# Three early routed slots instead of two in a fused mLSTM, dense layer and routed expert kernel

## The reference

```
y = mlstm(q, k, v, i_gate, f_gate, o_gate)        # 4 x 8 heads, 768 steps, head size 40
x = y.transpose(0, 2, 1, 3).reshape(3072, 320)
h = x @ w_in                                       # 320 x 2048
g = where(h >= 1, h, where(h <= -1, 0, (h + 1)**2 / 4))
x2 = g @ w_out                                     # 2048 x 320
logits = x2 @ w_gate                               # 8 experts
e = argmax(logits); gate = softmax(logits)[e]
out[e == i] = gate * (maximum(x2[e == i] @ w1[i], 0) @ w2[i])    # 320 x 1024, 1024 x 320
```

## Time and profile before

| | |
|---|---|
| median of 3 runs | 833.38 us (832.4 to 834.68) |
| the profiled execution | 833.21 us, its span 831.3 us |
| TensorE busy in the span | 767.5 us (92%) |
| VectorE, ScalarE, GpSimd busy | 593.1, 423.6, 317.3 us |
| mean granted TensorE clock | 0.984 of full |

### The profile page before, as it was taken

The page is one execution under the profiler, slowest core; times in us unless marked ns, Lnnn a source line. Parts: engine busy times, 40 slices in busy tenths (PEclk is TensorE's granted clock), DMA queues, the critical chain, the costliest instruction groups (busy, mean ns, idle before and its releaser), DMA issues.

```text
span 831.3 us, 17200 instructions
## 1 busy us (share of the span) xinstructions
PE 767.5 (92%) x5765; PEld 745.5 (90%) x5765; DVE 593.1 (71%) x1006; ACT 423.6 (51%) x649; POOL 317.3 (38%) x297
## 2 busy tenths in 40 slices
PE   2788999999999999999999999888659999999994
PEld 1788999999999999999999999888659999999994
DVE  4554868787887878888878786666376777776850
ACT  3024445454545455454646454554366666676751
POOL 3342543435454454434445444433232323231111
PEclk9999999999999999999999999999889999999998
DMA  7952222222232223222222202356965244627200
GB/s 222 297 153 74 76 90 75 89 79 96 85 99 79 100 92 94 75 89 74 89 74 89 84 6 71 110 163 207 327 212 173 104 133 159 219 77 227 83 20 5
DMA packets 41457, 97.05 MB, mean 117 GB/s; under 512 B 6937, under 2 KB 24481, under 8 KB 39754
## 3 DMA queue, kind: packets, MB, share of 16 engines
q1 hardware_dynamic: 37498, 87.46, 33.1%
q0 software_dynamic: 3920, 9.08, 3.6%
HBM read 105.63 MB, written 9.33 MB: 138 GB/s over the span
## 4 chain that ended last, share of the span: by engine, by line
PE 81%; DVE 7%; issue 4%; DMA 3%; ACT 3%; SPq 1%; POOL 0%; POOLq 0%; DVEq 0%; ACTq 0%
PE bank L1359 22%; PE bank L1371 21%; PE bank L1492 11%; PE bank L1439 7%; PE bank L1314 5%; PE bank L1305 3%; PE bank L1453 3%; PE bank L1322 2%; PE bank L1331 2%; DVE w_l L1045 2%; DVE w_l L1039 1%; DMA wTt<-in_w_outT 1%; DMA raw<-in_w 1%; ACT w_h L723 1%; PE bank L1385 1%
## 5 line engine op out<-in xcount | busy, mean ns | idle before, releaser
L539 POOL TENSOR_TENSOR g_t<-u_t,r_t 128x512 f32<-128x512 f32 x96 | 135.8, 1415 | 252.9 <-ACT u_t L689 252.9
L684 ACT ACTIVATE r_t<-bank,neg 128x512 f32<-128x512 f32 x96 | 66.0, 688 | 184.9 <-PE bank L1359 184.9
L1371 PE MATMUL bank<-wo_h,g_h 128*128 128x328 f32 x384 | 128.6, 335 | 5.9 <-DVE g_l L990 5.9
L1371 PE MATMUL bank<-wo_h,g_l 128*128 128x328 f32 x384 | 121.3, 316 | 0.0
L1371 PE MATMUL bank<-wo_l,g_h 128*128 128x328 f32 x384 | 121.2, 316 | 0.0
L984 DVE TENSOR_SCALAR u_t<-bank 128x512 f32<-128x512 f32 x96 | 66.1, 689 | 76.2 <-ACT r_t L684 46.9
L621 POOL DMA_INDIRECT out_x<-ob,idx_tok x31 | 37.7, 1217 | 171.5 <-ACT ob L759 167.5
L689 ACT ACTIVATE u_t<-u_t,half 128x512 f32<-128x512 f32 x96 | 69.6, 725 | 41.2 <-DVE u_t L984 40.1
L920 DVE TENSOR_TENSOR_SCAN W<-W,cst 128x512 f32<-128x512 f32 x48 | 83.6, 1745 | 3.8 <-DMA W<-decays 3.8
L1371 PEld LDWEIGHTS bank<-wo_h,g_h 128*128 128x128 f32 x384 | 73.4, 191 | 9.1 <-DVE g_l L990 6.6
L1359 PE MATMUL bank<-xT_h,wi_h 128*128 (+1 forms) x384 | 78.8, 287 | 1.6 <-issue 1.6
(11 more groups left out here) (231 smaller groups left out, 1943.1 us busy)
## 6 DMA issues: line engine op xcount, KB each, us to landing
raw<-in_w SPq DMA_DIRECT2D x12, 1280.0 KB
W<-decays SPq DMA_DIRECT2D x24, 512.0 KB, 5.0
raw<-in_w SPq DMA_DIRECT2D x12, 1024.0 KB
raw2n<-in_w SPq DMA_DIRECT2D x7, 1280.0 KB
raw1n<-in_w SPq DMA_DIRECT2D x7, 1024.0 KB
raw<-in_w SPq DMA_DIRECT2D x24, 256.0 KB
qG<-in_q SPq DMA_DIRECT2D x24, 180.0 KB
qT<-in_qt SPq DMA_DIRECT2D x48, 80.0 KB
```

The source lines that it names most:

```text
L539: pool.tensor_tensor(g_t[p % 2][:, :], u_t[p % 2][:, :], r_t[p % 2][:, :], ALU.add).then_inc(sm["g_done"], 1)
L684: act.activation(r_t[p % 2][:, :], bank_h[p % 2][:, :], ACT.Relu, bias=neg1[:, 0:1]).then_inc(sm["r_done"], 1)
L1371: mm = pe.matmul(bank_acc[tt][:, 0:DL], l[p % 4][:, c], r[:, f, :], start=f == 0 and a == 0, stop=f == NT1 - 1 and a == 2)
```

## The change

Slot kinds become PPPH, three times PPH, three times PH (before: five times PPH, twice PH); both have twelve P and seven H slots. `EARLY` is 3. The third early slot's gather and the reading of the early tokens move, and in the last block ScalarE's and VectorE's splits of slot 0's w1 come one piece later. Behind the last block the order on ScalarE, VectorE, TensorE and in SyncE's queue is written anew.

```diff
-KINDS = "PPH" * 5 + "PH" * 2
+KINDS = "PPPH" + "PPH" * 3 + "PH" * 3
-EARLY = 2
+EARLY = 3
@@ sync: last_stores, and behind the blocks
                 store_x2(t)
+                refill(1)
                 refill2(0)
...
-            load_routed(2)
-            load_routed2(2)
-            refill(1)
-            for s in range(2, NS):
+            load_routed(3)
+            refill(2)
+            load_routed2(3)
+            refill2(1)
+            for s in range(3, NS):
                 refill(s)
                 refill2(s - 1)
@@ gpsimd: body
-                    if not att and p == 5:
+                    gated(t, p)
+                    if not att and p == 1:
+                        table_rows(t, 1)
+                    if not att and p == 4:
                         for tt in range(2):
                             pool.wait_ge(x2_st[tt], 16 * t)
                         pool.wait_ge(sm["zrow"], 16)
                         pool.wait_ge(sm["list_done"], 1)
-                        gather(0)
-                    gated(t, p)
-                    if not att and p == 1:
-                        table_rows(t, 1)
-                    if not att and p == 6:
-                        gather(1)
+                    if not att and p in (4, 5, 6):
+                        gather(p - 4)
@@ scalar: body, tail, and behind the blocks (its first part)
-                    if not att and p in (4, 5):
-                        w1_high(0, p - 4)
+                    if not att and p in (5, 6):
+                        w1_high(0, p - 5)
...
                 w2_high(0, 0)
-                w2_high(0, 1)
...
             h_high(0, 0)
+            h_high(0, 1)
             w1_high(1, 0)
-            h_high(0, 1)
+            h_high(0, 2)
             w1_high(1, 1)
-            h_high(0, 2)
             h_high(0, 3)
             y_high(1)
+            w2_high(0, 1)
@@ vector: body and tail
-                        elif p == 5:
+                        elif p == 4:
                             early_tokens()
-                        if p in (5, 6):
-                            w1_low(0, p - 5)
+                        if p in (6, 7):
+                            w1_low(0, p - 6)
...
                 w2_low(0, 0)
-                w2_low(0, 1)
@@ tensor: body and tail
-                    if not att and p == 4:
+                    if not att and p == 3:
                         turn_table(1, bank_dc[:, 128:256], bank_dc[:, 256:384], 2 * EARLY)
...
                 turn_y(1)
                 second2(0, range(0, NT2 // 2))
-                first_wide(1, 0)
+                for p in range(4):
+                    first_wide(1, p)
+                turn_y(2)
                 turn_experts(2, bank_r[:, 256:384], HALVES)
-                for p in range(1, 4):
-                    first_wide(1, p)
-                second2(0, range(NT2 // 2, NT2 - 2))
+                second2(0, range(NT2 // 2, NT2))
+                for p in range(3):
+                    first_wide(2, p)
                 turn_table(2, bank_r[:, 0:128], bank_r[:, 128:256], HALVES)
-                second2(0, range(NT2 - 2, NT2))
+                first_wide(2, 3)
                 second2(1, range(0, NT2 - 2))
-                turn_y(2)
+                turn_y(3)
                 second2(1, range(NT2 - 2, NT2))
-                first2(2)
+                first2(3)
```

More of the change, by code:

```diff
@@ L809, in _ @@
             h_high(0, 0)
+            h_high(0, 1)
             w1_high(1, 0)
-            h_high(0, 1)
+            h_high(0, 2)
             w1_high(1, 1)
-            h_high(0, 2)
             h_high(0, 3)
             y_high(1)
+            w2_high(0, 1)
             h_high(1, 0)
-            w2_high(1, 0)
             h_high(1, 1)
-            w2_high(1, 1)
             h_high(1, 2)
             h_high(1, 3)
+            w1_high(2, 0)
+            y_high(2)
+            w1_high(2, 1)
             act.wait_ge(sm["list_done"], 1)
             out_gate(0)
-            w1_high(2, 0)
-            w1_high(2, 1)
-            y_high(2)
+            h_high(2, 0)
+            w2_high(1, 0)
+            h_high(2, 1)
+            w2_high(1, 1)
+            h_high(2, 2)
+            h_high(2, 3)
             w1_high(3, 0)
             w1_high(3, 1)
+            y_high(3)
+            out_gate(1)
             w2_high(2, 0)
             w2_high(2, 1)
+            w1_high(4, 0)
+            w1_high(4, 1)
+            w2_high(3, 0)
+            w2_high(3, 1)
             act.wait_ge(sm["list_done"], 2)
@@ L1187, in _ @@
             all_blocks(dve, body, ahead, tail, 2)
+            h_low(0, 1)
+            w1_low(1, 0)
+            h_low(0, 2)
             dve.wait_ge(sm["base_ready"], NBLK + 1)
@@ L1193, in _ @@
                                    cst[:, C_K128:C_K128 + AREA].unsqueeze(1).to_broadcast([P, E, AREA]), ALU.is_gt))
+            h_low(0, 3)
+            y_low(1)
+            w1_low(1, 1)
             then(dve.tensor_reduce(npair[:, :], cmp[:, :, 1:AREA:2], AX.X, ALU.add))
             then(dve.tensor_reduce(neven[:, :], cmp[:, :, 0:AREA:2], AX.X, ALU.add))
-            h_low(0, 1)
+            h_low(1, 0)
             then(dve.tensor_scalar(shift[:, E:2 * E], npair[:, :], 2.0, None, ALU.mult))
@@ L1215, in _ @@
             dve.tensor_copy(eb[:, :], ep[:, 0:1].to_broadcast([P, P])).then_inc(sm["eb_ready"], 1)
+            h_low(1, 3)
             then(dve.tensor_tensor(drow[:, :], shift[:, 1:2 * E + 1], shift[:, 0:2 * E], ALU.subtract))
@@ L1220, in _ @@
             then(dve.tensor_reduce(row[:, :], indr[:, :], AX.X, ALU.add))
-            y_low(1)
             then(dve.scalar_tensor_tensor(row[:, :], row[:, :], shift[:, 0:1], key[:, :], ALU.add, ALU.add))
@@ L1225, in _ @@
             dve.tensor_copy(rowi[:, :], row[:, :]).then_inc(sm["row_ready"], 1)
-            w1_low(1, 1)
-            h_low(1, 0)
+            w2_low(0, 1)
+            y_low(2)
+            w1_low(2, 0)
             dve.wait_ge(sm["tab_T"], 3)
-            three = bank_r[:, 256:281].rearrange("p (a b) -> p a b", b=5)
-            two = bank_r[:, 281:287].rearrange("p (a b) -> p a b", b=3)
-            then(dve.tensor_copy(e_int[:, 2:10].rearrange("p (a b) -> p a b", b=2), three[:, 1:5, 0:4:2]))
-            then(dve.tensor_copy(e_int[:, 10:12], two[:, :, 0]))
-            then(dve.tensor_copy(e_int[:, 12:17], three[:, :, 4]))
-            then(dve.tensor_copy(e_int[:, 17:19], two[:, :, 2]))
+            five = bank_r[:, 263:278].rearrange("p (a b) -> p a b", b=5)
+            three = bank_r[:, 278:287].rearrange("p (a b) -> p a b", b=3)
+            then(dve.tensor_copy(e_int[:, 3:9].rearrange("p (a b) -> p a b", b=2), five[:, :, 0:4:2]))
+            then(dve.tensor_copy(e_int[:, 9:12], three[:, :, 0]))
+            then(dve.tensor_copy(e_int[:, 12:16], bank_r[:, 262:278:5]))
+            then(dve.tensor_copy(e_int[:, 16:19], three[:, :, 2]))
             dve.tensor_tensor(e_new[:, EARLY:NS], e_int[:, EARLY:NS], e_int[:, EARLY - 1:NS - 1], ALU.not_equal).then_inc(sm["e_listed"], 1)
-            h_low(1, 1)
+            w1_low(2, 1)
+            h_low(2, 0)
             w2_low(1, 0)
-            h_low(1, 2)
+            h_low(2, 1)
             w2_low(1, 1)
-            h_low(1, 3)
+            h_low(2, 2)
             dve.wait_ge(sm["tab_T"], 4)
@@ L1243, in _ @@
             dve.tensor_copy(gate_slot[:, 2 * EARLY:HALVES], bank_r[:, 128 + 2 * EARLY:128 + HALVES]).then_inc(sm["list_done"], 1)
-            w1_low(2, 0)
-            w1_low(2, 1)
-            y_low(2)
+            h_low(2, 3)
             w1_low(3, 0)
             w1_low(3, 1)
+            y_low(3)
             w2_low(2, 0)
             w2_low(2, 1)
+            w1_low(4, 0)
+            w1_low(4, 1)
+            w2_low(3, 0)
+            w2_low(3, 1)
             for s in range(EARLY, NS):
@@ L1585, in _ @@
                     turn_y(s + 1)
-                if s > EARLY:
-                    second2(s - 1)
+                second2(s - 1)
                 if KINDS[s] == "H":
```

5 lines of the change are left out of this document (2 added, 3 removed).

## The result

The changed kernel took 830.70 us (826.99 to 833.15, 20 runs) where the kernel before, on the same chip, took 835.31 (830.9 to 839.59, 20 runs). The ratio is 0.9943 with a 95% interval of 0.9925 to 0.996: faster by 0.57%, some 4.7 us. The sign was forecast; of the 13.8 us only a third came, and 830.7 lies outside the range. The profiled executions, 830.88 and 833.21 us with spans of 829.1 and 831.3, are 2.3 us apart and not 4.6, because that of the kernel before is 2.1 us faster than its median.

A forecast was written before the change was run, and what follows sets the result against it. TensorE bounds it except at the block end (GpSimd's gathers) and 588 to 612 (single raw P buffer). Deciding product at 613.0 against 611.2 + 15.6 gains 13.8 us; 833.2 - 13.8 = 819.4 us, range 813.5 to 827.

The forecast's parts named there:

- the new wait of 3.9 us: In second2(0) at f = 4, TensorE waits 3.9 us for w2's second half split, plus 1.4 for slow clock.
- the remainder: After first_wide(4, 2) starts at 613.0: the same work with one P slot (15.6 us) less, TensorE bound.
- Part 1: End of the blocks: earlier table turn and gathers start slot 0's first product at 541.6, not 548.9; 7.3 us sooner.
- the trace shows 0.6 us, not 1.75: Block end: a gather issue near a VectorE split loses 0.6 us, rather than waiting out the 1.75 us split.
- if they do: Block end: if TensorE's waits for g_low of 0.4 and 1.5 us lower the clock, it costs another 1.4.
- the prediction's hardest reading: Block end: gathers near a split wait for its end (shared port pair); third gather and piece 7 end 1.2 us later.
- Part 2: Slot 0 to the list wait: TensorE goes on at 566.9 after a new wait; the list comes no sooner, about 570.6.
- Part 3: Third early slot: slot 2's loads skipped, slot 3's gather issued at 581.7, second2(1) ends at 588.9.
- I take 1.3, as less is in flight than before: TensorE's wait at turn_y(3) for slot 3's gathered rows: 1.3 us, from a possible 0 to 4.2.
- Part 4: Raw P buffer: slot 5's w1 issued at 598.6, landed 606.1; first_wide(4, 2) at 613.0 after some 7 us wait.
- Slot 4's w2 is still under way, so I take 7.5: Slot 5's w1 load: 7.5 us from issue to landing, between 6.9 alone and 10.4 in full traffic.
- transfers and gathers bind harder: Rival, 20 in 100: slower slot 3 gather, slot 3 load and slot 5 load; gain 6 to 10, time 823 to 827.

The follow-up runs named there:

- The experiment with the splits behind: Changed kernel with VectorE's splits of slot 0's w1 and w2 moved behind g_low(t, 7), none beside the third early gather; 833.2 us, ratio 0.9955.
- the three: Changed kernel with slot 4's w1 split and load ahead, slot 0's second w2 split half ahead of the list, gather 2 behind to_table; 822.12 us, ratio 0.9844.
- the w2 split: Changed kernel with the second half of slot 0's w2 split ahead of h_low(1, 0), not behind the final list; 827.32 us, ratio 0.9904.
- the first edit: Changed kernel with slot 4's w1 split ahead of slot 3's rows, out_gate(1) and slot 2's w2 split, refill(4) ahead of refill2(2); 821.33 us, ratio 0.9841.

## Why the prediction was wrong by its size

**What held.** The direction; the place that bounds the kernel (slot 5's w1 into the one P buffer), the new wait of 3.9 us with half clock behind it, the skipped loads of slot 2 (0.12 us at 561.10), a P slot at 15.6 us, and the remainder: 204.6 us from the deciding product to the end. The sum's form was right, with one wrong number in it: that product's start, 624.5 for 613.0.

**Part 1, 4.8 us late.** Slot 0's first product came at 546.41, not 541.6. The step that failed is "the trace shows 0.6 us, not 1.75". It took the duration of an issue that had begun in mid-split for the price of meeting one. Going along the path: piece 6's `gated` began 1.2 us later than forecast, which is this execution's own: its last store of x2 ahead of that place came at 514.62, in the kernel before at 513.20, and 513.20 and the usual 18.96 give 532.2, the forecast's 532.4. Gather 2's two issues then took 5.24 us, from 535.02 to 540.26, where the sum had 2.8 (2.4 more). Piece 7's `gated` took 0.4 more. TensorE waited 2.85 for it, not 1.5, and did its last piece at a mean clock of 0.59, 1.0 us more; that is the "if they do" of the forecast, which had 1.4. The length of the wait alone doesn't settle this term, as one kernel with a wait of 2.84 kept its clock at 1.00. These four, 1.2, 2.4, 0.4 and 1.0, make 5.0 for a delay of 4.8. The Trainium skill, "SBUF — State Buffer", section "SBUF: two separate sides", in the prediction's hardest reading (the issue waits for the split's end), agrees with these rows: the two issues ended 0.83 and 0.82 us behind their splits. The prediction's 1.2 us for that reading was half of the 2.4, as it counted one split where two met two issues. The experiment with the splits behind shows the cause: 0.97 and 0.95 us for the two issues, and the hold moved to the issue that met the split instead.

**Part 2, nothing more.** The list wait came at 571.61, 4.7 later than forecast: the same 4.8 us passed on.

**Part 3, 2.2 us.** "I take 1.3, as less is in flight than before" failed. The gather took 7.79 us, as the 8.0 of the earlier trace rows, because slot 4's w1 was in flight beside it: with that load out it landed in 3.6 us. TensorE's wait was 3.52.

**Part 4, 4.0 us.** "Slot 4's w2 is still under way, so I take 7.5" failed. The load took 11.45. The windows show 298 GB/s at a share of 0.93 from 573 to its issue and 318 at 0.95 until its landing. Loads saved by a skip aren't a free queue: whatever was next in SyncE's order took their place. In the eight other kernels with three early slots and all loads in, the landing was 9.15 to 12.2 us, so 7.5 was below all that any run showed at this place; why this execution had 11.45 and not 9.15 stays open, and some 2 of the 4.0 us may be chance. This is the rival "transfers and gathers bind harder", two of whose terms, 2.9 each, came as 2.2 and 4.0; together with Part 1's they leave the gain under its 6.

So 4.8 + 2.2 + 4.0 = 11.0 of the 11.5 us at the deciding product. All this is read from the profiled pair; by the medians 9.2 us of the forecast are missing.

**What the prediction did not ask.** It listed that the load waits for slot 4's split, this for slot 2's w2 split and `out_gate(1)`, and took the order as given. That order cost more than any mis-sized term: moving one split ahead of the others gave 9.4 us. With it the change would have come out at 821.3, near the 819.4 forecast, but by luck, for the mis-sized terms would have stood.

**What stays open.** Why the edits don't add. Cutting 2.9 MB out of the three gave 5.4 us by the medians, so traffic has a part in it, but the trace of that kernel is of its slowest execution and shows no shorter landing. That the 3.4 us of the w2 split, taken alone, vanish in the traffic beside the first edit is argued, not shown. Open too is what makes the same load land in 9.15 us in one trace and in 12.2 in another.

## What to carry to other kernels

When work is added ahead of a stage that is fed by a single buffer, first find which instruction frees that buffer and put it ahead of all that nobody waits for; here that was worth twice the change. Read the end of a row against the ends on the other engine, not its duration: a wait that began late looks like a small price. And where a load is skipped, look at what the queue sends instead before booking a shorter landing.

## What the runs showed of the hardware

- An indirect transfer's issue on GpSimd that begins while a two-input VectorE operation of 1.75 us runs ends 0.82 to 0.85 us after that operation, in the five rows read here, and takes 0.95 to 0.97 with none beside it. One that began 0.20 us ahead of such an operation took 0.97. A two-input elementwise operation on GpSimd of 1.30 us ended 1.13 after the split and took 2.57; VectorE's own split behind it took 2.56 instead of 1.48.
- Half the clock followed TensorE's waits of 2.85 us (mean 0.59 over the next 3.0 us) and 3.87 us (0.50 over 2.4 us) in the changed kernel; behind a wait of 2.84 us in another kernel the clock stayed at 1.00.
- The landing of a gather of 128 rows was 3.6 us at a DMA share of 0.48 and 7.8 at 1.03. A w1 load of 1.6 MB landed in 8.6 us at 0.85, and in anything from 9.15 to 12.2 us at 0.94 to 1.02, so the share doesn't tell the landing time.
- In all twelve kernels with three early slots the span's end came 204.4 to 205.6 us behind the third piece of slot 5. That product started between 612.13 (span 816.6) and 626.85 (span 831.3), so the start of one product told the time to 1.2 us.
